# Linear attention into a mixture of experts: state products over four quarters of the array, logits beside the turn of x, w1a in 31 pieces

## Time and profile before

| what | value |
|---|---|
| median of 3 runs | 558.56 us (557.83 to 561.11) |
| profiled execution, its own time | 553.72 us |
| its span | 551.9 us |
| mean granted TensorE clock of the span | 0.982 |
| TensorE busy | 505.7 us (92% of the span) |
| DMA moved | 107.91 MB |

### The profile page before, as it was taken

The page is one execution under the profiler, slowest core; times in us unless marked ns, Lnnn a source line. Parts: engine busy times, 40 slices in busy tenths (PEclk is TensorE's granted clock), DMA queues, the critical chain, the costliest instruction groups (busy, mean ns, idle before and its releaser), DMA issues.

```text
span 551.9 us, 13507 instructions
## 1 busy us (share of the span) xinstructions
PE 505.7 (92%) x4845; PEld 300.0 (54%) x4846; DVE 277.2 (50%) x449; ACT 187.2 (34%) x345; POOL 257.0 (47%) x216
## 2 busy tenths in 40 slices
PE   4899999998887476699999999999999999999995
PEld 4787778785566334345454544545454454545442
DVE  1765756564710589664454646373737233242431
ACT  0122222213000545764546363645452232222210
POOL 1211221220100014544586878777777766656543
PEclk9999999999998789989999999999999999999998
DMA  8899999877999999805534462222232333333420
GB/s 269 309 340 417 368 338 408 309 303 263 387 422 411 420 410 409 299 21 210 191 115 142 176 196 42 42 41 52 40 60 37 56 49 49 44 55 41 49 29 2
DMA packets 32502, 107.91 MB, mean 196 GB/s; under 512 B 11583, under 2 KB 12847, under 8 KB 28240
## 3 DMA queue, kind: packets, MB, share of 16 engines
q1 hardware_dynamic: 18288, 92.89, 44.0%
q0 software_dynamic: 14176, 14.49, 14.1%
HBM read 93.87 MB, written 29.43 MB: 223 GB/s over the span
## 4 chain that ended last, share of the span: by engine, by line
PE 86%; DVE 4%; DMA 4%; issue 3%; ACT 1%; POOL 1%; SPq 0%; DVEq 0%; POOLq 0%
PE ps L968 51%; PE ps L699 5%; PE ps L951 5%; PE ps L652 4%; PE ps L693 4%; DMA w_region<-moe_w 3%; PE ps L841 3%; PE ps L684 3%; PE ps L819 3%; PE ps L706 2%; PE ps L877 2%; PE ps L673 1%; PE ps L666 1%; PE ps L728 1%; DMA w_region<-chunks 1%
## 5 line engine op out<-in xcount | busy, mean ns | idle before, releaser
L968 PE MATMUL ps<-w_region,s_region 128*128 (+1 forms) x1320 | 294.8, 380 | 1.1 <-ACT s_region L1147 1.1
L968 PEld LDWEIGHTS ps<-w_region,s_region 128*128 128x128 f16 x1320 | 127.1, 98 | 144.8 <-issue 2.6
L1570 DVE SCALAR_TENSOR_TENSOR s_region<-ps,s_region 128x1024 f16<-128x1024 f32 x55 | 67.3, 1223 | 147.7 <-ACT s_region L1147 147.7
L1147 ACT ACTIVATE s_region<-ps 128x1024 f16<-128x1024 f32 x55 | 56.3, 1023 | 182.0 <-PE ps L951 181.9
L603 POOL DMA_INDIRECT out<-s_region,rec_region x41 | 55.9, 1363 | 52.9 <-DVE s_region L1599 49.8
L609 POOL DMA_INDIRECT out<-s_region,rec_region x42 | 67.9, 1616 | 16.2 <-issue 11.9
L597 POOL DMA_INDIRECT rec_region<-records,idx x55 | 59.9, 1090 | 24.0 <-issue 16.4
L540 POOL TENSOR_TENSOR s_region<-w_region,s_region 128x512 f32<-128x512 f32 x22 | 22.9, 1042 | 89.6 <-PE ps L706 73.7
L951 PEld LDWEIGHTS ps<-s_region,sw_region 128*128 (+1 forms) x440 | 29.4, 98 | 15.3 <-issue 2.7
L1599 DVE TENSOR_SCALAR s_region<-ps,rec_region,y_scale 128x512 f32<-128x512 f32 x42 | 33.7, 803 | 5.8 <-PE ps L968 4.6
L951 PE MATMUL ps<-s_region,sw_region 128*128 128x128 f16 x440 | 34.1, 220 | 2.0 <-issue 2.0
(11 more groups left out here) (243 smaller groups left out, 563.2 us busy)
## 6 DMA issues: line engine op xcount, KB each, us to landing
w_region<-moe_w SPq DMA_DIRECT2D x11, 2048.0 KB, 10.0
w_region<-chunks SPq DMA_DIRECT2D x34, 512.0 KB, 6.7
w_region<-moe_w SPq DMA_DIRECT2D x26, 512.0 KB, 16.0
w_region<-moe_w SPq DMA_DIRECT2D x12, 1024.0 KB, 9.1
s_region<-moe_w SPq DMA_DIRECT2D x4, 2048.0 KB, 16.0
sw_region<-chunks SPq DMA_DIRECT2D x12, 512.0 KB, 7.6
s_region<-moe_w SPq DMA_DIRECT2D x2, 1024.0 KB, 8.3
w_region<-moe_w SPq DMA_DIRECT2D x1, 1536.0 KB, 7.9
```

The source lines that it names most:

```text
L968: last = nc.tensor.matmul(bank[6 + r], h[:, r, f, :], w2b_parts[:, bass.ds(o, 1), part, f, :].rearrange("p e m -> p (e m)"), start=(first ...
L1147: nc.scalar.activation(h_hi[:, r, :, :].rearrange("p c t -> p (c t)").rearrange("p (a n) -> p a n", a=2), ps[:, 2 + 2 * r:4 + 2 * r, :], A ...
L1570: nc.vector.scalar_tensor_tensor(out=h_lo[:, r, :, :].rearrange("p c t -> p (c t)").rearrange("p (a n) -> p a n", a=2), in0=ps[:, 2 + 2 * ...
```

## The change

**State products.** The output of the attention now lies in two banks, one for even and one for odd heads, each with 256 columns. A state product of head i (rows 64 i of the array) writes to partition half `half`, so that four consecutive products lie on the four 64 x 64 quarters (rows 0 or 64, columns 0 or 64) instead of two on the diagonal. This permutes the channels of x; phi, w1a and the output decays are permuted on the host to match.

**Logits.** The product that sums the partial logits is done one chunk later (of t - 2) and stands right behind the turn of x; so does ScalarE's copy of it. The wait for the state moves from before the turn to before that product. The partial logits get two SBUF buffers. Partial logits now share a bank with the odd heads' output, and logits, group maxima and state share another; waits that keep these apart are added, and a group's maximum and shift come behind the state on VectorE.

**w1a.** 31 pieces of 512 KB, one or two behind each `load_kv(g)` from g = 3 on, instead of 16 larger ones. The bytes are the same.

**GpSimd's loop** over the decays is written out.

```diff
-        Y, ST, T_X, LG = range(4, 8)
+        Y, T_X, ST = 4, 6, 7
+        y_of = [bank[Y + i][:, 0:2 * P] for i in range(2)]
+        y_all = ps[:, Y:Y + 2, 0:2 * P]
+        parts_at = bank[Y + 1][:, 2 * P:3 * P]
+        den_at = bank[Y + 1][:, 400:402]
+        state_at = bank[ST][:, 0:NP * D]
+        rows_at = bank[ST][:, NP * D:NP * D + SL]
+        turned_at = bank[ST][:, NP * D + SL:NP * D + SL + P]
+        spread_at = bank[ST][:, NP * D + SL + P:NP * D + 2 * SL + P]
...
-            HALF = UNIT // 2
-            def w1a_half(e, half):
-                words = slice(half * HALF, (half + 1) * HALF)
-                sp.dma_start(w1a_home[e][:, words], w1a[e, :, words]).then_inc(w1a_early, 16)
-            def late_w1a_words(first, last):
-                sp.dma_start(late_w1a[:, first:last], w1a[E - 1, :, first:last]).then_inc(w1a_early, 16)
+            def w1a_quarter(e, q):
+                words = slice(q * UNIT // 4, (q + 1) * UNIT // 4)
+                to = late_w1a if e == E - 1 else w1a_home[e]
+                sp.dma_start(to[:, words], w1a[e, :, words]).then_inc(w1a_early, 16)
...
-                more = (g - 2) * 2 * E // (NT - 3)
-                for half in range(ahead, more):
-                    if half < 2 * (E - 1):
-                        w1a_half(half // 2, half % 2)
-                    elif half == 2 * (E - 1):
-                        late_w1a_words(0, HALF)
-                    else:
-                        late_w1a_words(HALF, LATE)
+                more = (g - 2) * (4 * E - 1) // (NT - 3)
+                for q in range(ahead, more):
+                    w1a_quarter(q // 4, q % 4)
                 ahead = more
...
+            def logit_parts_of(t):
+                pe.wait_ge(x_t_ready, t + 1)
+                if t > 0:
+                    pe.wait_ge(parts_kept, t)
...
+            def logit_rows(t):
+                pe.wait_ge(parts_kept, t + 1)
+                for g in group_ending(t):
+                    pe.wait_ge(max_diag_ready, g + 1)
+                for g in group_ending(t - 1):
+                    pe.wait_ge(cols_shifted, g + 1)
+                if t > 0:
+                    pe.wait_ge(logits_kept, t)
+                nc.tensor.matmul(rows_at, logit_parts[t % 2], stack, start=True, stop=True).then_inc(logits_done, 1)
...
             def outputs(b, c):
+                t = b * NC + c
+                if t > 0:
+                    pe.wait_ge(parts_kept, t)
                 if c > 0:
-                    for n in range(NP):
-                        for i in range(2):
-                            part = slice(i * D, (i + 1) * D)
-                            nc.tensor.matmul(bank[Y][part, n * P:(n + 1) * P], state[part, n, :],
-                                             qt_in[(b * NC + c) % QK_DEPTH][part, n, :],
-                                             start=(n == 0), stop=False, skip_group_check=True)
-                pe.wait_ge(v_decayed, b * NC + c + 1)
-                pe.wait_ge(probs_ready, b * NC + c + 1)
+                    for m in range(2):
+                        for half in range(2):
+                            for i in range(2):
+                                rows, n = slice(i * D, (i + 1) * D), 2 * m + half
+                                nc.tensor.matmul(y_of[i][half * D:(half + 1) * D, m * P:(m + 1) * P], state[rows, n, :],
+                                                 qt_in[t % QK_DEPTH][rows, n, :],
+                                                 start=(m == 0), stop=False, skip_group_check=True)
+                pe.wait_ge(v_decayed, t + 1)
+                pe.wait_ge(probs_ready, t + 1)
+                for m in range(2):
+                    for i in range(2):
+                        for half in range(2):
+                            n = 2 * m + half
+                            h = 2 * n + i
+                            last = nc.tensor.matmul(y_of[i][half * D:(half + 1) * D, m * P:(m + 1) * P],
+                                                    v_dec[c % 2][:, h * D:(h + 1) * D], probs[c % 2][:, i, n, :],
+                                                    start=(c == 0 and m == 0), stop=(m == 1), skip_group_check=True)
+                last.then_inc(y_ready, 1)
...
+                t = b * NC + c
+                if t > 1:
+                    pe.wait_ge(logits_kept, t - 1)
...
-                        logit_parts_of(before_b, before_c)
-                        if c > 0:
-                            pe.wait_ge(state_ready, b * (NC - 1) + c)
-                        turn_x(before_b, before_c)
-                    t = b * NC + c
+                    logit_parts_of(t - 1)
+                    turn_x(t - 1)
+                    if c > 0:
+                        pe.wait_ge(state_ready, b * (NC - 1) + c)
+                    if t > 1:
+                        logit_rows(t - 2)
+                    outputs(b, c)
+                    if c < NC - 1:
+                        update(b, c)
                     for g in group_ending(t - 1):
+                        pe.wait_ge(logits_kept, t - 1)
                         turn_max(g)
                     for g in group_ending(t - 2):
+                        pe.wait_ge(logits_kept, t - 1)
                         spread_max(g)
-                    outputs(b, c)
-                    if c > 0 or b > 0:
-                        logit_rows(before_b, before_c)
-                    if c < NC - 1:
-                        for g in group_ending(t - 1) + (group_ending(t - 2) if c == 0 else []):
-                            pe.wait_ge(max_diag_ready, g + 1)
-                        for g in group_ending(t - 2) + (group_ending(t - 3) if c == 0 else []):
-                            pe.wait_ge(cols_shifted, g + 1)
-                        update(b, c)
...
-                            den_sums(g, t)
+                            den_sums(g, t + 1)
             scores(0, 0)
             for b in range(B):
                 sequence_products(b)
-            logit_parts_of(B - 1, NC - 1)
-            turn_x(B - 1, NC - 1)
-            logit_rows(B - 1, NC - 1)
+            logit_parts_of(NT - 1)
+            logit_rows(NT - 2)
+            turn_x(NT - 1)
+            logit_rows(NT - 1)
...
-            def keep_chunk(g):
-                act.wait_ge(parts_done, g + 1)
-                nc.scalar.activation(logit_parts, bank[LG][:, 0:P], ACT.Copy).then_inc(parts_kept, 1)
+            def keep_logits(t):
+                act.wait_ge(logits_done, t + 1)
+                nc.scalar.activation(logits[:, t, :], rows_at, ACT.Copy).then_inc(logits_kept, 1)
+            def keep_chunk(t):
+                act.wait_ge(parts_done, t + 1)
+                if t > 1:
+                    act.wait_ge(logits_done, t - 1)
+                nc.scalar.activation(logit_parts[t % 2], parts_at, ACT.Copy).then_inc(parts_kept, 1)
...
-                act.wait_ge(x_turned, g + 1)
-                nc.scalar.activation(x_home(g), bank[T_X][:, :], ACT.Copy).then_inc(x_kept, 1)
-                act.wait_ge(logits_done, g + 1)
-                nc.scalar.activation(logits[:, g, :], bank[LG][:, P:P + SL], ACT.Copy).then_inc(logits_kept, 1)
+                if t == NT - 1:
+                    keep_logits(t - 1)
+                act.wait_ge(x_turned, t + 1)
+                nc.scalar.activation(x_home(t), bank[T_X][:, :], ACT.Copy).then_inc(x_kept, 1)
+                if 0 < t < NT - 1:
+                    keep_logits(t - 1)
...
+            keep_logits(NT - 1)
+            exp_slots(NG - 1)
             keep_den(NG - 2)
-            exp_slots(NG - 1)
             keep_den(NG - 1)
...
                     for g in group_ending(t - 1):
+                        find_max(g)
+                    keep_x_t(b, c)
+                    for g in group_ending(t - 1):
+                        dve.wait_ge(col_max_turned, g + 1)
+                    for g in group_ending(t - 2):
+                        dve.wait_ge(max_spread, g + 1)
+                    if c < NC - 1:
+                        keep_state(b, c)
+                    for g in group_ending(t - 1):
                         join_max(g)
                     for g in group_ending(t - 2):
                         shift_cols(g)
-                    keep_x_t(b, c)
-                    for g in group_ending(t):
-                        find_max(g)
-                    if c < NC - 1:
-                        keep_state(b, c)
```

More of the change, by code:

```diff
@@ L462, in _ @@
                     sp.dma_start(gates[:, :, E:2 * E], w_noise.rearrange("(c p) e -> p c e", p=P)).then_inc(small_full, 16)
-            assert ahead == 2 * E
+            assert ahead == 4 * E - 1
             def load_w2b(o):
@@ L564, in _ @@
             pool.wait_ge(v_decayed, 2)
-            for c in range(2, NC):
-                decay_chunk(0, c)
-            with pool.Fori(1, B) as b:
-                for c in range(NC):
-                    decay_chunk(b, c)
+            for t in range(2, NT):
+                decay_chunk(t // NC, t % NC)
```

(46 more changed lines are left out.)

69 lines of the change are left out of this document (37 added, 32 removed).

## The result

| | before | after |
|---|---|---|
| median | 558.24 us (557.83 to 561.11, 4 runs) | 550.23 us (549.34 to 551.57, 4 runs) |
| profiled execution, and its span | 553.72 us, 551.9 us | 549.43 us, 547.7 us |
| scores of the last chunk begin | 122.84 us | 117.75 us |

The medians lie 8.0 us apart, and the ratio of the runs is 0.9848 (0.9806 to 0.9889), about 1.5% faster. I had forecast 14 us. The spans of the two profiled executions differ by 4.2 us only; what that is worth is taken up with the first experiment.

A forecast was written before the change was run, and what follows sets the result against it. TensorE was taken to bound the attention, with loads close behind. TensorE's terms gave 15.3 us, the loads at 395 GB/s 13.3; rounded up to 14, 558.56 became 544.5 us, range 541 to 553.5.

The forecast's parts named there:

- TensorE's sum: Attention on TensorE: a middle chunk falls from 5.13 to 4.32 us, attention ends 15.3 us earlier if nothing else binds.
- The Trainium skill's rule of the row groups: State products: weight loads overlap running products only where row groups differ, so no gain; forecast took 0.44 us instead.
- The loads as second limit: DMA in the attention: 37.65 MB at 17 to 120 us bound a faster TensorE, leaving 13.3 us gain.
- I take 395: Attention's loads: 395 GB/s assumed between 374 and 410, last scores at 111.0 us, 11.8 us earlier.
- the very lower bound: Attention's loads: 374 GB/s, as in its first 40 us at share 1.00, last scores at 116.4 us.
- the first rival: Attention: loads bind at their low rate, 374 GB/s; gain 6.4 + 1.5, 8 us less, 550.5; chance 15%.
- the main sum: Whole kernel: TensorE's 15.3 us against the loads' 13.3, rounded up to a 14 us gain, 544.5 us.
- the fourth rival: Attention's loads: smaller pieces slow the one queue, at 335 GB/s the kernel is 3.5 us slower, 562; chance 4%.
- Single loads: Attention: a chunk's load lands in 6.9 us with 7.8 us of room, so not late until the rate is.
- Carry-over: After the attention: later stages, loads included, move forward whole, so the gain carries over in us, 558.56 - 14.
- Waits at group ends: Logits' sum at four group ends waits for maximum and shift on VectorE: 1 us in all.
- Pieces of 512 KB: w1a loads in the attention: 15 more issues on SyncE cost nothing.

The follow-up runs named there:

- the first experiment: The kernel before, unchanged, recorded once more: its profiled execution took 558.52 us, where the first recording took 553.72 us.

## Why the prediction was right in kind and too large

- **TensorE's sum: right.** State products 0.59 (0.58 forecast), logits summed without a gap, update begun 0.93 behind the score products, last scores 109.5 with the loads out of the way (109.0). The Trainium skill's rule of the row groups ("TensorE: Matmul & The Clock Gate", "The mechanism"), by which I had worked out that 1.02 would stay, does not agree with this trace: two of four 64 x 64 quarters have the same rows, and the group takes 0.59.
- **The loads as second limit: right; the rate in it: wrong.** The step that failed is "I take 395". The window rows give 376, 386 and 349 GB/s. Up to 117 us that is 40 x 0.376 + 39 x 0.386 + 21 x 0.349 = 37.4 MB in 100 us, 374 GB/s, the very lower bound. That bound put the last scores at 116.4 and the program at 550.5; measured were 117.75 and 550.23. So the first rival, which I had given 15%, is the case, and its mark stood in the text: scores wait for DMA while DMA reads under 380. That 550.5 came out to 0.3 us is partly chance, since the last scores came 5.1 us earlier and not the 6.4 of that sum. And 550.23 lies in the range because its upper end, 553.5, had been set to take in this rival; the main sum gave 544.5.
- **Why 395 was wrong.** I split the difference between 374 and the 410 of a later stage, on the ground that even pieces would keep the queue full. But the earlier trace rows had share 1.00 at 374 already: the queue was not short of work, each packet was slow, and even pieces hardly raised the rate there (376 GB/s from 17 to 57 us). One slow stretch has a cause that the runs show, the loads with 32-byte rows. They were in the kernel before too, where 33 to 40 us read 298 GB/s at share 0.99, hidden while TensorE needed 5.13 us a chunk. That is also below the 335 that the fourth rival took as the lowest rate at full share.
- **Single loads: late, though I wrote that they would not be "until the rate is".** I had 7.8 us of room for a load that landed after 6.9. With TensorE faster, a chunk's load landed after 7.8 us (8.2 to 8.6 for the other group of buffers), and those in the chain after up to 9.5. With w1a out of the way it was 5.4. Rate and delay rose and fell together in these runs. No run gave k and v a third buffer, which would have changed the delay that TensorE sees and not the bytes, so that rival stands untested.
- **Carry-over: right within what can be told.** Last scores moved by 5.1 us (first recordings) and 5.6 (second ones, 123.9 to 118.3), and w1a's first product by 6.2 and 6.4 us. The medians moved by 8.0 and 7.2. Where the rest of 1 to 2 us lies is not shown. The clock behind the attention, 0.94 and 0.85 for the same kernel, differs enough from one execution to the next to cover it.
- **Waits at group ends: too large.** I took 1 us for four of them ahead of the last scores. In after the weight load of the sum of the logits stood idle there in two places, 0.6 us in all, and the profile names no engine for it; the one wait for a shift, 0.4 us, stands behind them, at 123.9 us. **Pieces of 512 KB:** they did not make the gain, as I had said; that they cost nothing is not shown, since both recordings with 16 pieces had a shorter attention (95.9 and 95.1 us against 97.9 and 98.0).
- **Open:** why packets are slow in other stretches at nearly full share (324 GB/s from 74 to 80 us and 319 from 102 to 108 in after; with 16 pieces 74 to 80 us read 387 and 396); what the missing k does by itself; and how much of 8 us the quarters, and how much the logits' new place, would bring alone, since no run undid only one of them.

## What to carry to other kernels

Before making the busiest engine faster, work out the next limit from the rate measured in that same stretch; where the DMA share is 1.00 already, do not forecast with a better rate of another stage unless something that slows the packets is taken away. When loads become the bound, look for small loads with short rows and for data nobody reads: taking both out of the stretch gave 4.6 us here with 31 pieces, and the traces give what they show of it to the small loads; with 16 pieces nothing was gained. Count from a fixed point inside the stretch, since the first 20 us of a recording can hide or feign 1 us. And record the kernel before twice when two profiles are to be subtracted.

## What the runs showed that I had not expected

- A DMA share of 1.00 stood beside 275 and beside 407 GB/s: the share tells that packets are in flight, not that they are fast. With two loads of 1024 rows of 32 bytes in all among them, 33 to 40 us read 329 to 339 GB/s in five recordings; without, 398 to 411 in four.
- Four quarters of 64 x 64 take sixteen records in 0.59 to 0.61 us in either order of issue, also where the same quarter comes twice in the order before the other diagonal is issued.
- One kernel, two recordings: 553.72 and 558.52 us, with a mean granted clock of 0.94 and 0.85 between 120 and 235 us. Inside the attention the granted clock was 1.00 but for two places. A gap of 2.33 us in TensorE's work (w1a spread further) was followed by about 3 us at 0.50. So was one of 1.32 us (other order of quarters, idle up to 17.02 us), in this window:

```profile
17.00:21.00 4.00, 3.98 (x44) 3.14 (x46) 1.40 (x3) 0.88 (x2) 0.46 (x1) 0.57 0.84 278
```

The waits for loads of up to 1.34 us in the change, and one of 1.93 us in the kernel with 16 pieces and late gates (idle up to 74.22 us), had no such effect. So the length of a single gap does not tell, in these traces, whether the clock falls.
